# Value block means from plain rows of 128 keys, in place of means over overlapping spans of 96 keys

## What is computed

```python
k_sum = k.reshape(B, H, nb, block, D).max(axis=3)
v_sum = v.reshape(B, H, nb, block, D).mean(axis=3)        # block = 32, nb = 24
scores_l = scale * q @ k^T, kept where |i - j| < 16
scores_s = scale * q @ k_sum^T + log(block)
a = softmax(concat([scores_l, scores_s]))
out = a @ concat([v, v_sum])
```

## Time and profile before

| | |
|---|---|
| median of three runs | 1066.01 us (1064.84 to 1074.94) |
| the profiled execution | 1066.68 us |
| its span in the trace | 1064.9 us |
| granted TensorE clock, mean | 0.925 of full |
| busy: PE, PEld, DVE | 84%, 69%, 64% of the span |
| busy: ACT, POOL | 29%, 27% of the span |
| read from memory, written | 79.57 MB, 19.51 MB |
| DMA queue q1 (SP's) | 61.63 MB |

### The profile page before, as it was taken

The page is one execution under the profiler, slowest core; times in us unless marked ns, Lnnn a source line. Parts: engine busy times, 40 slices in busy tenths (PEclk is TensorE's granted clock), DMA queues, the critical chain, the costliest instruction groups (busy, mean ns, idle before and its releaser), DMA issues.

```text
span 1064.9 us, 21948 instructions
## 1 busy us (share of the span) xinstructions
PE 898.2 (84%) x7342; PEld 733.7 (69%) x7343; DVE 681.6 (64%) x1998; ACT 305.5 (29%) x626; POOL 285.1 (27%) x390
## 2 busy tenths in 40 slices
PE   4899999915899999999996233999898989998995
PEld 3787878714688888888885122868686867687884
DVE  5757576575666666666665567777777768674440
ACT  2544454505322212222221003223232322223330
POOL 5733344101012111111220005050515151414501
PEclk9999999956899999999998655999999999999998
DMA  9676675915011111111110123414141414155100
GB/s 195 122 160 135 133 153 100 280 50 185 11 51 40 50 40 40 40 40 40 40 50 20 24 71 119 159 51 169 50 169 54 165 61 159 61 204 172 32 29 30
DMA packets 45631, 99.94 MB, mean 94 GB/s; under 512 B 6736, under 2 KB 19072, under 8 KB 45440
## 3 DMA queue, kind: packets, MB, share of 16 engines
q1 hardware_dynamic: 26816, 61.63, 19.8%
q0 software_dynamic: 8064, 26.46, 7.9%
q10 hardware_dynamic: 10688, 11.01, 4.9%
HBM read 79.57 MB, written 19.51 MB: 93 GB/s over the span
## 4 chain that ended last, share of the span: by engine, by line
PE 69%; DVE 18%; issue 4%; POOL 3%; ACT 2%; DMA 2%; DVEq 0%; ACTq 0%; SPq 0%; POOLq 0%
PE bank L777 27%; PE bank L898 11%; PE bank L912 9%; PE bank L689 4%; PE bank L670 3%; PE bank L848 3%; DVE w_low L1649 2%; PE bank L730 2%; PE bank L707 2%; PE bank L801 2%; PE bank L679 2%; POOL slot_hot L635 2%; DVE xl L1653 1%; DVE ge L1517 1%; ACT xh L1042 1%
## 5 line engine op out<-in xcount | busy, mean ns | idle before, releaser
L1404 DVE SCALAR_TENSOR_TENSOR bank<-y,wg 128x512 f32<-128x512 f32 x200 | 132.0, 723 | 2.9
L635 POOL TENSOR_SCALAR slot_hot<-iota_l,mlo 128x128 bf16<-128x128 f32 x96 | 72.0, 766 | 214.7 <-DVE mlo L1622 214.7
L898 PE MATMUL bank<-xh,w_high 128*128 128x384 f32 x256 | 94.3, 368 | 16.1 <-DVE hl L1639 8.9
L777 PE MATMUL bank<-w_high,hh 128*128 x200 | 83.2, 416 | 13.2 <-DVE hl L1393 13.2
L777 PE MATMUL bank<-w_high,xh 128*128 x200 | 82.7, 414 | 10.7 <-DVE gates L1386 10.7
L592 POOL DMA_INDIRECT y_rows<-y,sidx x25 | 25.0, 998 | 243.2 <-DVE bank L1404 243.2
L898 PE MATMUL bank<-xh,w_low 128*128 128x384 f32 x256 | 88.1, 344 | 0.0
L898 PE MATMUL bank<-xl,w_high 128*128 128x384 f32 x256 | 87.9, 344 | 0.0
L1042 ACT ACTIVATE hh<-bank 128x512 fp32r<-128x512 f32 x50 | 27.1, 595 | 203.1 <-PE bank L801 203.1
L1418 DVE TENSOR_SCALAR y<-bank,gates 128x512 f32<-128x512 f32 x25 | 18.8, 751 | 101.1 <-PE bank L777 101.1
L912 PE MATMUL bank<-w_high,hh 128*128 128x512 f32 x192 | 82.3, 429 | 0.0
(11 more groups left out here) (285 smaller groups left out, 1932.5 us busy)
## 6 DMA issues: line engine op xcount, KB each, us to landing
w_landed<-in_moe_w SPq DMA_DIRECT2D x16, 2048.0 KB, 10.5
va<-in_v_win SPq DMA_DIRECT2D x16, 585.0 KB, 6.4
raw_w<-in_moe_w SPq DMA_DIRECT2D x4, 2048.0 KB, 11.3
k_raw<-in_k SPq DMA_DIRECT2D x16, 384.0 KB, 9.1
q_eye<-in_q ACTq DMA_DIRECT2D x16, 384.0 KB, 7.4
x_rows<-x ACTq DMA_DIRECT2D x12, 384.0 KB, 10.2
wg<-in_moe_w_gate SPq DMA_DIRECT2D x1, 2048.0 KB, 25.8
x_rows<-x SPq DMA_DIRECT2D x4, 387.0 KB, 7.2
```

The source lines that it names most:

```text
L635: last = g.tensor_scalar(slot_hot[:, j, :], iota_l[:, :], mlo[:, j:j + 1], None, ALU.is_equal)
L777: last = mm(ps, lhs[a][:, c, :], rhs[b](c), start=c == 0 and t == 0, stop=c == n - 1 and t == 2)
L898: last = mm(bank[fc % 2][:, 0:CAP], w[:, q % 2, c, f], a[:, c, :], start=c == 0 and t == 0, stop=c == KC - 1 and t == 2)
L1404: stt(bank[6 + e % 2][:, :], y[:, 0:DM], 1.0, wg2[:, e, :], ALU.mult, ALU.mult, accum_out=y[:, DM + e:DM + e + 1]).then_inc(l2_out, 1)
```

## The change

A second form of the values is made on the host and loaded: `v_rows`, for each pair 128 partitions x 6 chunks x 128 numbers (partition p of chunk c is key 128c+p, both heads side by side), 384 KB for a pair. It lands in `vrows`, two buffers used in turn, with semaphores of their own. `average` becomes 128 x 6 x 24. The means of a pair are six matmuls with a stationary operand of 128 x 24 and a moving one of 128 x 128. `va` stays as it is for the values product; the wait for its load moves from `means` to `values`. GpSimd builds `average` with two selections in place of four.

SP loads the rows of pairs 0 and 1 right behind the first values. Inside the loop, `refill_rows` for pair hp+2 stands at the head of iteration hp, ahead of `refill_k` and `refill_v` of the same iteration, and behind `refill_v` (and for hp = 2 the store of L436) of the iteration before. Its own wait asks for the means of pair hp.

```diff
+            def load_rows(b, m):
+                sp.dma_start(vrows[m % 2][:, :, :], v_rows[bass.ds(b, 1), m, :, :, :, :].rearrange("o p c h d -> (o p) c (h d)")
+                             ).then_inc(vr_loaded[m % 2], 16)
+
             load_k(0, 0)
             load_k(0, 1)
             load_v(0, 0)
+            load_rows(0, 0)
+            load_rows(0, 1)
             sp.dma_start(wg[:, :, :], w_gate.rearrange("(c p) e -> p c e", p=P)).then_inc(small_loaded, 16)
...
                         sp.wait_ge(pv_done, UNITS * b + PU * (hp + 1))
                         load_v(nb, nhp)
 
+                    def refill_rows(cb_, m):
+                        sp.wait_ge(means_made, HP * b + m - 1)
+                        load_rows(cb_, m % HP)
+
+                    if hp < HP - 2:
+                        refill_rows(b, hp + 2)
                     with sp.If(b < B - 1):
                         nb = nc.s_assert_within(b + 1, 0, B - 1, skip_runtime_bounds_check_because="b < B - 1 here")
+                        if hp >= HP - 2:
+                            refill_rows(nb, hp + 2)
                         refill_k(nb, hp)
                         refill_v(nb, hp)
...
             chain(g.memset(avg, 1.0 / BLOCK))
-            pick([[QB, NQ], [-BLOCK, NB]], -WINDOW, 1)
-            pick([[-QB, NQ], [BLOCK, NB]], WINDOW + BLOCK - 1, -1)
-            pick([[-2, NQ], [1, NB]], 0, 0)
-            pick([[2, NQ], [-1, NB]], 1, 0)
+            chain(g.affine_select(out=avg, in_=avg, compare_op=ALU.is_ge, fill=0.0, base=0, pattern=[[P, QT], [-BLOCK, NB]], channel_multiplier=1))
+            chain(g.affine_select(out=avg, in_=avg, compare_op=ALU.is_ge, fill=0.0, base=BLOCK - 1, pattern=[[-P, QT], [BLOCK, NB]], channel_multiplier=-1))
...
             def means(b, m, n):
-                pe.wait_ge(vw_loaded[m % HP], 16 * (b + m // HP + 1))
+                pe.wait_ge(vr_loaded[m % 2], 16 * (HP // 2 * b + m // 2 + 1))
...
-                for j in range(NQ):
-                    last = mm(bank[4 + (n + 1) % 2][WK:PW, MEAN0:MEAN0 + 2 * D], average[:, j, :], va[m % HP][0:WK, :, j, 0:D],
-                              start=j == 0, stop=j == NQ - 1)
+                for c in range(QT):
+                    last = mm(bank[4 + (n + 1) % 2][WK:PW, MEAN0:MEAN0 + 2 * D], average[:, c, :], vrows[m % 2][:, c, :],
+                              start=c == 0, stop=c == QT - 1)
                 last.then_inc(means_made, 1)
 
             def values(b, n):
 
                 hp, i = n // PU, n % PU
                 if i == 0:
+                    pe.wait_ge(vw_loaded[hp % HP], 16 * (b + hp // HP + 1))
                     pe.wait_ge(vsum_done, HP * b + hp + 1)
```

More of the change, by code:

```diff
@@ L110, in val, with two_layers_of_experts @@
     return k + x.c if x.c else k
-def two_layers_of_experts(nc, queries, k, v_win, modality_id, w_gate, modality_bias, w1, w2,
+def two_layers_of_experts(nc, queries, k, v_win, v_rows, modality_id, w_gate, modality_bias, w1, w2,
                           w_gate2, w1b, w2b, out):
@@ L245, in two_layers_of_experts @@
         vw_loaded = [sem(f"vw_loaded{i}") for i in range(HP)]
+        vr_loaded = [sem(f"vr_loaded{i}") for i in range(2)]
         pads_ready = sem("pads_ready")
@@ L289, in two_layers_of_experts @@
         span_mask = sa("span_mask", [P, PW])
-        average = sa("average", [WK, NQ, NB])
+        vrows = [sa(f"v_rows{i}", [P, QT, 2 * D]) for i in range(2)]
+        average = sa("average", [P, QT, NB])
         vst = [sa(f"vst{i}", [PW, 2, D]) for i in range(2)]
@@ L531, in _ @@
             avg = average[:, :, :]
-            pick = lambda pattern, base, per: chain(g.affine_select(out=avg, in_=avg, compare_op=ALU.is_ge, fill=0.0, base=base,
-                                                                    pattern=pattern, channel_multiplier=per))
             chain(g.memset(avg, 1.0 / BLOCK))
-            pick([[QB, NQ], [-BLOCK, NB]], -WINDOW, 1)
-            pick([[-QB, NQ], [BLOCK, NB]], WINDOW + BLOCK - 1, -1)
-            pick([[-2, NQ], [1, NB]], 0, 0)
-            pick([[2, NQ], [-1, NB]], 1, 0)
+            chain(g.affine_select(out=avg, in_=avg, compare_op=ALU.is_ge, fill=0.0, base=0, pattern=[[P, QT], [-BLOCK, NB]], channel_multiplier=1))
+            chain(g.affine_select(out=avg, in_=avg, compare_op=ALU.is_ge, fill=0.0, base=BLOCK - 1, pattern=[[-P, QT], [BLOCK, NB]], channel_multiplier=-1))
             for t in va:
@@ L1731, in laid_out @@
     laid["v_win"] = rows
+    laid["v_rows"] = v.reshape(B, HP, 2, QT, P, D).transpose(0, 1, 4, 3, 2, 5)
     laid["moe2_w_gate"] = _np.asarray(inputs["moe2_w_gate"]).T
     return laid
-_INS = ['q', 'k', 'v_win', 'moe_modality_id', 'moe_w_gate', 'moe_modality_bias', 'moe_w1', 'moe_w2',
+_INS = ['q', 'k', 'v_win', 'v_rows', 'moe_modality_id', 'moe_w_gate', 'moe_modality_bias', 'moe_w1', 'moe_w2',
         'moe2_w_gate', 'moe2_w1', 'moe2_w2']
```

## The result

The changed kernel takes 1111.53 us (median of 4 runs, 1108.23 to 1115.69) against 1066.13 for the kernel before: ratio 1.0395, 95% interval 1.0356 to 1.0435. The profiled execution took 1115.69 us, its span is 1113.9 us.

What follows compares the result with a forecast made beforehand. TensorE was taken to bound attention, the means (L689) leading with 17.0% of the chain. Terms: +2.5 at pair 2, -19.6 matmuls, +51.7 waits, +5 clock, together +39.6 us: 1106 profiled, 1105 median; range 1076 to 1128.

Steps and rivals of the forecast that it cites:

- The stand-in: Landing of rows read from key loads right behind the values in the kernel before; twelve waits, 51.7 us in sum.
- with the store: Two of twelve pairs, a store of L436 between values load and means; TensorE would wait 6.3 us each.
- with logits: Three of twelve pairs, logits of the gate between values load and means; TensorE would wait 2.3 us each.
- plain pairs: Seven of twelve pairs, neither store nor logits between values load and means; TensorE would wait 4.6 us each.
- The clock: TensorE's granted clock falling behind long waits: 1.55 us for about a third of nine, 5 us; possible 0 to 24.
- Nine waits: TensorE's forecast waits for rows of 4.6 or 6.3 us, each priced between 0 and 2.7 us for the clock.
- The start: First burst of loads: 0.79 MB net more, pair 2's rows landing at about 32.2 us, pair 2 shifted +2.5 us.
- The matmuls: Means on TensorE, six matmuls fewer: 1.40 us saved a pair, 2.66 at the first, 23.7 us over 16 pairs.
- The rival in which everything queues: Clock falls at all nine waits, query loads slow too, rows land in 10 us: 1120 to 1135; chance 0.13.
- The faster rival: Transfers quicker than the stand-in, values at 4 us and rows at 5: sum -13, 1053 us; chance 0.05.
- break-even: In the faster rival, given as a plain wait of 1.8 us, each microsecond off being worth 9 us.
- Theory B: In the follow-up expectations: the additional 6.3 MB cost the time wherever issued; 1066 or more with rows asked for sooner.

Runs made afterwards that it cites:

- the matmuls alone: Changed kernel with rows loaded for pairs 0 and 1 only, every later pair's means made from these; 0.987 of the kernel before.
- the filled kernel: Changed kernel with twelve discarded matmuls ahead of TensorE's wait for rows; 1.0365 of the kernel before, then 1.0324 beside the changed kernel's 1.0368.
- rows sooner: Changed kernel with each pair's rows asked for one iteration of SP's loop sooner, pair 2's ahead of the loop; 1.0017 of the kernel before.
- the loads alone: Changed kernel's row loads in their places, but means made as before by twelve matmuls over the old values, rows unused; 1.0003 of the kernel before.
- four buffers: Changed kernel with four row buffers, rows asked for a batch ahead with the keys, and ahead of the values in the first burst; 1.0004 of the kernel before.
- keys ahead of rows: Changed kernel with SP's refill of keys moved ahead of the refill of rows; 1.0634 of the kernel before.

## Why the prediction was right, and where its sizes were off

**The mechanism and the sign.** The step that said that the rows, held by the values refill ahead of them, are asked for only two steps before their use and land too late is shown from three sides: the wait is in twelve pairs of the trace with the rows' transfer as releaser; it goes when the rows are asked for sooner (1.0017), and it grows when one more transfer is put ahead (1.0634). That the loads themselves cost next to nothing in their place is shown by the run without their wait (1.0003).

**The stand-in.** The keys of the kernel before, taken for the rows of the one after, gave a landing 8.8, 10.9 and 9.9 us behind the values. The rows took 8.2 us from issue in the median, and were issued 0.6 to 0.9 us behind the values (1.4 with the store between). By kind: with the store 7.3 and 8.0 against 6.3 forecast; with logits 2.0, 1.5 and 2.4 against 2.3; plain pairs 5.5, 4.2 and 4.0 against 4.6. But four of the seven plain pairs waited only 1.0 to 2.3 us. The quick key load of the earlier trace rows was not an outlier to bound with, it stood in one of these places. What they share is the order against ScalarE's query load. In pairs 3, 7 and 11 the rows were issued ahead of it, by 0.25 to 1.7 us, and landed in 6.7, 4.9 and 5.8 us; where it was ahead, without a store, they took 7.6 to 9.1, except in pair 13 (5.2, the query load 0.12 us ahead). The second trace of the changed kernel has 7.1, 5.6 and 5.9 in the same three pairs and 6.7 to 10.3 in the others without a store. The key load of the earlier trace rows was 0.7 us ahead of the query load; the one of 137.57, taken for all plain pairs, was 0.1 behind it. No run changed this order alone, so it is read from the traces and not tested. The sum came to 42.1 in place of 51.7.

**The clock.** This is the term that was mis-sized: 5 us, with an upper end of 24, against 21.9 measured. Nine waits were rated by 1.55 us at one chance in three. Of these nine, six were followed by a fall, and it cost 1.5 to 2.6 us each, 11.8 in sum. Every wait of 4.0 us or more was followed by doubled durations, the five of the loop and the one of pair 2; of those between 2.0 and 2.4 us three were (pairs 3, 6 and 14) and one wasn't (2.12 in pair 11). The rest was in places that the term left out: pair 2 (2.7) and two of the pairs with logits, whose products ran at half clock too (4.3 and 4.6). The Trainium skill's page "TensorE: Matmul & The Clock Gate", section "HAM oscillation — how this bites in real kernels", whose kernel has the clock fall at each wait for a transfer, was put at 14 us in the prediction; it is nearer than the share I took, though four of the twelve waits here brought no fall.

**The start.** +4.2 us at pair 2 against +2.5: its rows came at 33.9, forecast 32.2. The sum had them in the first burst, behind nothing but bytes. In fact their own wait, for the means of pair 0 (done at 17.0), held them, and they landed 16.7 us after this issue:

```profile
17.16 0.37 SPq L414 DMA_DIRECT2D v_rows<-in_v_rows  x1
```

The first means did shrink, to 2.73 us.

**The matmuls.** -1.31 us a pair on TensorE (2.80 to 1.49) against -1.40. "If nothing else changed ... 1043" holds as worded, but other things change: with the waits taken away the gain is 14 us, not 23.7, because GpSimd's spans, VectorE's results and the queries are next. In the changed kernel this didn't show, as the waits for rows hid it.

So 1105 for 1111.5 came from a sum whose waits were 10 us too long and whose clock was 17 us too short, and which left out 4.6 us of smaller waits that went; that these nearly cancel is luck. The rival in which everything queues (1120 to 1135) had the clock about right. The faster rival failed on its condition: the rows never landed within 5 us of the values' issue; the quickest took 5.5. (Its break-even is also misstated: by its own terms a plain wait of 2.2 us gives no change and one of 1.0 us a gain of 1%, not 1.8.) Theory B of the expectations, that transfers in general are too many, was right in one point that no run of the changed kernel could show, that queries are late once the rows are early.

## What to carry to other kernels

A load is as early as the last wait ahead of it in its queue's program, not as its own wait. Before adding one, read from the trace when the instruction in front of it issues and how long the next transfer behind took to land: this gave the size of the waits to within a quarter here. And when an engine's work is cut, price the cut by taking the work out alone, since the next chains (here GpSimd, VectorE and the query loads) may keep part of it, 10 of 24 us here. A landing time taken as a stand-in holds for the place that it was read from, with the same loads of other queues issued ahead of it.

## What the runs showed of the hardware

A wait of TensorE can cost more than its length. Behind each of the six waits of 4.0 us or more in the changed kernel the clock was at its half level for 4 to 6 us; a wait of 3.08 us in the run with the matmuls alone was followed by durations of 1.87 in place of 1.04 us. The length alone doesn't decide: 2.03 us in pair 6 were followed by a fall and 2.12 in pair 11 not, and in the second trace of the filled kernel neither were 3.39 us that came right behind discarded matmuls. Filling the waits with discarded matmuls shortened the phase.

A copy of one number per partition on GpSimd (L578, the row index for a gather), beside four subtractions of VectorE in a row, takes either 1.1 or 4.5 us. In the timeline of the kernel before it is

```profile
250.58 1.11 POOL L578 COPY gidx<-idx 128x1 int32<-128x1 int32 x1 [12.12 <-DVE gates L1386]
```

and in that of the changed kernel

```profile
297.00 4.52 POOL L590 COPY gidx<-idx 128x1 int32<-128x1 int32 x1 [12.13 <-DVE gates L1399]
```

where TensorE then waits 4.1 us for the gather, and 2.6 us of the 49.0 are lost after attention. It isn't a property of the kernel: the changed kernel's second trace has the short form. Of all thirteen traces six have the long one (the changed kernel's first, rows sooner, the loads alone, both filled ones, four buffers) and seven the short one. From the first expert matmul to the end of the span it is 847.4 to 853.1 us in the six and 842.9 to 845.3 in the seven, except 849.5 with keys ahead of rows. VectorE's four subtractions last 4.6 us from 0.15 us before the copy begins (in the run with rows sooner), so the long form ends with them. The Trainium skill, page "SBUF — State Buffer", section "SBUF: two separate sides", has VectorE with two SBUF inputs and GpSimd reading SBUF exclude each other for a whole instruction; by it the copy would pass after one subtraction, as the short form does. The long one shows that it can also wait for all four. What decides was not tried, and that the copy waits for VectorE is read from the times that coincide. It may be part of the spread of some 10 us between executions of one kernel.
